# Moving the first expert's weight split into the last chunks of the block loop, with a new order for the last second products and for one 2 MB load

## The reference

```python
kv  = softmax(k, over tokens).T @ v                     # per batch and head
x   = softmax(q, over channels) @ kv                    # [4608, 512]
h   = x @ w_in                                          # [4608, 2048]
y   = (h - tanh(h)) @ w_out                             # [4608, 512]
logits = norm(y) @ norm(expert_emb).T / tau             # 8 experts
e, gate = argmax(logits), softmax(logits)[argmax]
out = gate * (relu(y @ w1[e]) @ w2[e])                  # w1 512x1024, w2 1024x512 for each expert
```

## Time and profile before

| what | value |
|---|---|
| time before, median of 3 runs | 1449.97 us (1447.04 to 1451.49) |
| the profiled execution's own time | 1449.26 us |
| its span, first to last instruction | 1447.2 us |
| mean granted TensorE clock | 0.998 of full |
| block loop ends, expert loop begins | about 967 us from the span's start |
| DMA over the span | 90.58 MB, mean 63 GB/s |

### The profile page before, as it was taken

How to read it: one execution, slowest core, us unless ns; L and a number is a source line. 1 busy time by engine, 2 the same in 40 slices (tenths; PEclk the granted TensorE clock), 3 DMA queues, 4 the chain that set the end, 5 groups by cost and what they waited for, 6 DMA issues and landing times.

```text
span 1447.2 us, 27386 instructions
## 1 busy us (share of the span) xinstructions
PE 1413.6 (98%) x8120; PEld 1218.9 (84%) x8121; DVE 904.7 (63%) x1755; ACT 765.1 (53%) x1574; POOL 396.6 (27%) x346
## 2 busy tenths in 40 slices
PE   6999999999999999999999999999999999999997
PEld 5788888888888888888888888878788888888886
DVE  7986788886688888578888666676314213342111
ACT  5886576666666676657666666663313223242211
POOL 4522253433244443325343323231000000000000
PEclk9999999999999999999999999999999999999999
DMA  9631021221011222002121002035411411411110
GB/s 214 179 93 61 1 72 30 68 50 49 1 47 43 55 50 50 25 1 72 30 68 26 23 1 81 0 103 192 136 44 61 139 44 40 160 36 46 44 38 29
DMA packets 140226, 90.58 MB, mean 63 GB/s; under 512 B 116504, under 2 KB 120856, under 8 KB 139936
## 3 DMA queue, kind: packets, MB, share of 16 engines
q1 hardware_dynamic: 133344, 69.27, 18.5%
q0 software_dynamic: 5840, 18.92, 3.4%
q10 hardware_dynamic: 880, 0.55, 0.1%
HBM read 69.80 MB, written 21.28 MB: 63 GB/s over the span
## 4 chain that ended last, share of the span: by engine, by line
PE 88%; DVE 5%; issue 2%; ACT 2%; DMA 1%; POOL 1%; ACTq 0%; SPq 0%; DVEq 0%; POOLq 0%
PE ps L554 26%; PE ps L555 26%; PE ps L556 25%; PE ps L632 2%; PE ps L752 2%; PE ps L654 1%; PE ps L724 1%; PE ps L643 1%; PE ps L638 1%; DVE gs L1054 1%; PE ps L674 1%; PE ps L625 1%; DMA out<-osb,xrow 1%; PE ps L597 1%; DMA xrow<-scratch 1%
## 5 line engine op out<-in xcount | busy, mean ns | idle before, releaser
L1461 POOL TENSOR_TENSOR g_lo<-gs,g_hi 128x384 fp32r<-128x384 f32 x192 | 199.0, 1037 | 575.4 <-ACT g_hi L851 575.2
L554 PE MATMUL ps<-x_hi,wi_hi 128*128 128x384 f32 x768 | 277.9, 362 | 2.2 <-DVE x_lo L1108 1.1
L555 PE MATMUL ps<-x_lo,wi_hi 128*128 128x384 f32 x768 | 260.0, 339 | 0.0
L556 PE MATMUL ps<-x_hi,wi_lo 128*128 128x384 f32 x768 | 259.9, 338 | 0.0
L841 ACT ACTIVATE usq<-ps 128x384 f32<-128x384 f32 x192 | 94.1, 490 | 290.4 <-PE ps L556 289.8
L554 PE MATMUL ps<-wo_hi,g_hi 128*128 128x512 f32 x576 | 228.4, 397 | 4.4 <-POOL g_lo L1461 3.0
L555 PE MATMUL ps<-wo_lo,g_hi 128*128 128x512 f32 x576 | 229.1, 398 | 0.0
L556 PE MATMUL ps<-wo_hi,g_lo 128*128 128x512 f32 x576 | 227.4, 395 | 0.0
L965 ACT ACTIVATE hb<-ps 128x512 f32<-128x512 f32 x74 | 44.3, 599 | 308.4 <-PE ps L556 303.9
L1051 DVE SCALAR_TENSOR_TENSOR gs<-gs,ps 128x384 f32<-128x384 f32 x192 | 105.8, 551 | 152.0 <-ACT gs L846 151.4
L1054 DVE TENSOR_TENSOR gs<-gs,usq 128x384 f32<-128x384 f32 x192 | 176.7, 920 | 0.0
(11 more groups left out here) (213 smaller groups left out, 2682.0 us busy)
## 6 DMA issues: line engine op xcount, KB each, us to landing
w_raw<-w SPq DMA_DIRECT2D x10, 2048.0 KB, 9.0
xrow<-scratch SPq DMA_DIRECT2D x36, 257.0 KB, 2.7
k_sb<-k SPq DMA_DIRECT2D x60, 144.0 KB, 3.4
q_sb<-q SPq DMA_DIRECT2D x60, 144.0 KB, 3.0
v_sb<-v SPq DMA_DIRECT2D x60, 144.0 KB, 3.4
in_raw<-w_in SPq DMA_DIRECT2D x8, 512.0 KB, 6.8
out_raw<-w_out SPq DMA_DIRECT2D x8, 512.0 KB, 6.0
scratch<-pad_d SPq DMA_DIRECT2D x8, 257.0 KB, 4.4
```

The source lines that it names most:

```text
L554: mm(out_, a_hi, b_hi, start=first, stop=False)
L555: mm(out_, a_hi, b_lo, start=False, stop=False)
L556: return mm(out_, a_lo, b_hi, start=False, stop=last)
L1461: G.tensor_tensor(g_lo[:, (s - 1) % 3], gs[:, (s - 1) % 2], g_hi[:, (s - 1) % 3].bitcast(F32), ALU.subtract).then_inc(glo_ready, 1)
```

## The change

Five edits go together. (1) The first expert's w1 is split by column halves: piece 0 is columns 0 to 511 of all four rows, piece 1 the rest (`first_piece`, `first_raw`). The left half is split inside the loop: ACT's copy ahead of slot 43 (`SUPER - 5`), and the subtraction on DVE in two parts of 128 x 1024, ahead of slots 43 and 45 (`left_lo`); it raises `left_ready`, on which alone `hidden(0, half 0)` waits. The right half's copy stands ahead of slot 46. (2) The second products of the last two chunks issue the six passes on `g_hi` first and wait for `g_lo` only then. (3) `g_lo` of the very last chunk is computed by DVE (`last_lo`). (4) The last-but-one block's third scatter is issued in the same slot as the other two, and so ahead of `g_lo` of chunk 46 on POOL. (5) SP issues the load of w2 only when the rows of 11 blocks are stored.

```diff
--- before.py
+++ after.py
@@ -291,7 +291,7 @@
     first_step, first_known, second_known, tab_step, tab_ready, pads_stored = (
         sem(x) for x in ("first_step", "first_known", "second_known", "tab_step", "tab_ready", "pads_stored"))
     raw_in = [sem("w1_raw_in"), sem("w2_raw_in")]
-    b_hi_done, w_ready = sem("b_hi_done"), sem("w_ready")
+    b_hi_done, w_ready, left_ready = sem("b_hi_done"), sem("w_ready"), sem("left_ready")
     row_in = [sem(f"row_in{i}") for i in range(4)]
     out_stored = [sem(f"out_stored{i}") for i in range(4)]
     t_ready, thi_ready, tlo_ready, hid_ready, relu_done = (
@@ -379,6 +379,17 @@
         if i < 2:
             return w1_raw[:, 2 * i:2 * i + 2].rearrange("p c n -> p (c n)")
         return w2_raw[:, 4 * (i - 2):4 * (i - 1)].rearrange("p c n -> p (c n)")
+
+    def first_piece(w_1, w_2, i):
+
+        if i < 2:
+            return w_1[:, 0, :, 512 * i:512 * (i + 1)]
+        return w_2[:, 0, 4 * (i - 2):4 * (i - 1)]
+
+    def first_raw(i):
+        if i < 2:
+            return w1_raw[:, :, 512 * i:512 * (i + 1)]
+        return w2_raw[:, 4 * (i - 2):4 * (i - 1)]
 
     def startup(engine, part, chunk_, piece_, emb_):
 
@@ -488,6 +499,7 @@
         row0 = sp.value_load(e_row[0:1, 0:1], min_val=0, max_val=ROWS - KNOWN * P)
         for j in range(KNOWN):
             sp.dma_start(xrow[:, j], scratch[ds(row0 + j * P, P), :]).then_inc(row_in[j], 16)
+        sp.wait_ge(rows_stored, 16 * GPB * (NBLK - 1))
         load_w2(e0)
 
         def entry(t, col, hi):
@@ -575,6 +587,18 @@
             c = s % FC1
             if isinstance(m, int) and m == 0 and s < FC1 and s % 2 == 0:
                 pe.wait_ge(wo_lo_done, s // 2 + 1)
+            if isinstance(m, int) and m * SUPER + s >= NCH - 2:
+                pe.wait_ge(ghi_ready, done(m, s))
+                for g in range(GPB):
+                    t = slice(g * P, (g + 1) * P)
+                    mm(y_ps[g], g_hi[:, s % 3, t], wo_hi[:, c], start=False, stop=False)
+                    mm(y_ps[g], g_hi[:, s % 3, t], wo_lo[:, c], start=False, stop=False)
+                pe.wait_ge(glo_ready, done(m, s))
+                for g in range(GPB):
+                    t = slice(g * P, (g + 1) * P)
+                    last = mm(y_ps[g], g_lo[:, s % 3, t], wo_hi[:, c], start=False, stop=c == FC1 - 1)
+                last.then_inc(l2_done, 1)
+                return
             pe.wait_ge(glo_ready, done(m, s))
             for g in range(GPB):
                 if c == 0:
@@ -735,6 +759,9 @@
 
             if hf == 0:
                 pe.wait_ge(tlo_ready, t + 2)
+            if isinstance(t, int) and t == 0 and hf == 0:
+                pe.wait_ge(left_ready, 1)
+            elif hf == 0 or isinstance(t, int) and t == 0:
                 pe.wait_ge(w_ready, e * 2 + 1)
             pe.wait_ge(relu_done, t * 2 + (hf + 1))
             f = slice(512 * hf, 512 * (hf + 1))
@@ -932,17 +959,16 @@
         def hi_of_first(i):
 
             act.wait_ge(raw_in[i // 2], 16)
-            nc.scalar.copy(expert_piece(w1_hi, w2_hi, i, 0), expert_raw(i)).then_inc(b_hi_done, 1)
+            if i < 2:
+                act.wait_ge(h_ready, done(3, SUPER - 5 + 4 * i))
+            nc.scalar.copy(first_piece(w1_hi, w2_hi, i), first_raw(i)).then_inc(b_hi_done, 1)
 
         def t_split(t, j):
             act.wait_ge(t_ready, t + 1)
             nc.scalar.copy(t_hi[:, j % 2], ps[:, 0].rearrange("p (c n) -> p c n", c=DC)).then_inc(thi_ready, 1)
 
-        def first_hi():
-            t_split(0, 0)
-            hi_of_first(1)
-
-        walk(act, slot, {SUPER - 2: lambda: hi_of_first(0), SUPER - 1: first_hi})
+        walk(act, slot, {SUPER - 5: lambda: hi_of_first(0), SUPER - 2: lambda: hi_of_first(1),
+                         SUPER - 1: lambda: t_split(0, 0)})
 
 
 
@@ -1238,10 +1264,27 @@
         def lo_of_first(i):
 
             dve.wait_ge(b_hi_done, i + 1)
-            last = V.tensor_tensor(expert_piece(w1_lo, w2_lo, i, 0), expert_raw(i),
-                                   expert_piece(w1_hi, w2_hi, i, 0).bitcast(F32), ALU.subtract)
+            last = V.tensor_tensor(first_piece(w1_lo, w2_lo, i), first_raw(i),
+                                   first_piece(w1_hi, w2_hi, i).bitcast(F32), ALU.subtract)
             if i % 2:
                 last.then_inc(w_ready, 1)
+
+        def left_lo(b):
+
+            dve.wait_ge(b_hi_done, 1)
+            d = slice(2 * b, 2 * b + 2)
+            last = V.tensor_tensor(first_piece(w1_lo, w2_lo, 0)[:, d], first_raw(0)[:, d],
+                                   first_piece(w1_hi, w2_hi, 0)[:, d].bitcast(F32), ALU.subtract)
+            if b == 1:
+                last.then_inc(left_ready, 1)
+
+        def last_lo():
+
+            c = SUPER - 1
+            dve.wait_ge(glo_ready, done(3, c, -1))
+            dve.wait_ge(ghi_ready, done(3, c))
+            V.tensor_tensor(g_lo[:, c % 3], gs[:, c % 2], g_hi[:, c % 3].bitcast(F32),
+                            ALU.subtract).then_inc(glo_ready, 1)
 
         e_used, e_turn, e_below, e_is, e_other, e_no = (x[:] for x in early)
         one_e = cst[0:1, C_ONE:C_ONE + 1].broadcast_to([1, E])
@@ -1267,7 +1310,7 @@
             V.tensor_copy(e_first[:], e_used[:, 0:1])
             V.tensor_scalar(e_row[:], e_used[:, 0:1], float(REGION), float(P), ALU.mult, ALU.add).then_inc(first_known, 1)
 
-        walk(dve, slot, {EARLY: choose_first})
+        walk(dve, slot, {EARLY: choose_first, SUPER - 5: lambda: left_lo(0), SUPER - 3: lambda: left_lo(1)})
         def t_split(t, j):
             dve.wait_ge(thi_ready, t + 1)
             V.tensor_tensor(t_lo[:, j % 2], ps[:, 0].rearrange("p (c n) -> p c n", c=DC),
@@ -1279,7 +1322,7 @@
                 V.tensor_tensor(h_lo[:, j % 2, 4 * b:4 * b + 4], ps[:, 3 + b].rearrange("p (c n) -> p c n", c=4),
                                 h_hi[:, j % 2, 4 * b:4 * b + 4].bitcast(F32), ALU.subtract).then_inc(hlo_ready, 1)
 
-        lo_of_first(0)
+        last_lo()
         t_split(0, 0)
         lo_of_first(1)
         route_part("tail_squares", NBLK - 1, 0)
@@ -1456,7 +1499,7 @@
 
         def lo(m, s):
 
-            if within(m, s, -1):
+            if within(m, s, -1) and not (isinstance(m, int) and m * SUPER + s == NCH):
                 pool.wait_ge(ghi_ready, done(m, s, -1))
                 G.tensor_tensor(g_lo[:, (s - 1) % 3], gs[:, (s - 1) % 2], g_hi[:, (s - 1) % 3].bitcast(F32),
                                 ALU.subtract).then_inc(glo_ready, 1)
@@ -1482,8 +1525,18 @@
                 if g == 0:
                     pool.wait_ge(dest_ready, j + 1)
                     hold(pool)
-                G.indirect_dma_start(scratch, bass.IndirectOffsetOnAxis(ap=dest[:, g:g + 1].bitcast(U32), axis=0),
-                                     yrow[:, g], None).then_inc(rows_stored, 16)
+                if isinstance(j, int) and j == NBLK - 2:
+                    if g == 1:
+                        scatter(1)
+                        scatter(2)
+                    elif g == 0:
+                        scatter(0)
+                else:
+                    scatter(g)
+
+        def scatter(g):
+            G.indirect_dma_start(scratch, bass.IndirectOffsetOnAxis(ap=dest[:, g:g + 1].bitcast(U32), axis=0),
+                                 yrow[:, g], None).then_inc(rows_stored, 16)
 
 
         def embeddings(i):
```

## The result

The changed kernel takes 1453.7 us in the median of 8 runs (1452.28 to 1454.79), the kernel before 1450.34 (1447.04 to 1452.12). The ratio is 1.0025, 95% interval 1.0015 to 1.0034: 3.4 to 3.6 us slower, inside the range and on the side that was forecast (+2.0). The span of the profiled execution is 1450.8 us, 3.6 more than before.

A forecast was written before the change was run, and what follows sets the result against it. PE was taken as the bound, busy 1413.6 of 1447.2 us. -2.95 (stalls gone) +3.6 (new wait) +1.3 (clock) = +1.95, say +2.0, on the median 1450.0 gave 1452.0 us; range 1447.3 to 1456.0.

The forecast's parts named there:

- Parts 1 to 3: Chunk 46 to hidden(0, half 0): halves cost nothing, new pass order and g_lo on DVE remove three stalls, -2.95 us.
- The scatters: POOL's scatters beside DVE's left parts: delay taken as 0, at most 0.8 us.
- The scatter's landing: Third scatter, from 958.58: lands after 4.8 us at 963.4, and only then SP issues w2.
- Part 4, the new wait: Before tail_logits: w2 takes 9.0 us, ACT's copies come late, PE idles 3.6 us, logits start 0.65 later.
- Part 5, the clock: At the 24 logits products: clock falls earlier after the idle time, some run at 1.2 GHz, +1.3 us.
- the recovery: Clock's recovery after the logits products: taken as nothing, bounds -1.4 to +0.7 us against before.
- Half of the bound: Clock cost in the logits products: bounds 0 and 2.7 us, of which half less a little was taken.
- What is absorbed later: Row load behind the table, PE's wait at 998.77: absorbs up to 0.55 us of what only PE loses.
- C: Logits: idle PE drops to 1.2 GHz before all 24 products, through hidden(1, half 0); +4.05, 1454 to 1457 us; chance 0.18.
- A: Before the logits: scatter and w2 land early, wait 0 to -2.1, clock around 0; 1448 to 1450.5 us; chance 0.22.
- B: ACT's wait off the path, w2 landed by 968.8: full gain -2.95 or -4.35, 1445.6 to 1447 us; chance 0.05.
- D: Last chunks: halves don't fit or POOL is held up, +0.8 us, 1452.8; chance counted within the forecast's 0.55.

The follow-up runs named there:

- e8: Changed kernel with both DVE left parts ahead of slot 43; one execution at granted clock 0.95, 1455.63 us, not compared.
- e6: Kernel before with only the w1 column halves, the other four edits undone; 1451.59 us beside 1449.77, ratio 1.0009 to before.
- e3: Changed kernel with 16 extra unused 512-column products on PE ahead of tail_logits; 1451.98 us beside 1448.64, ratio 1.0021 to before.
- e1: Changed kernel without SP's wait before loading w2; 1450.36 us beside 1448.64, ratio 1.0013 to before.
- e2: Kernel before with only SP's wait before loading w2 added; 1452.96 us beside 1448.64, ratio 1.0027 to before.
- e5: e4 with SP's load of the second expert's w1 put behind the table; 1452.88 us beside 1449.77, ratio 1.0019 to before.
- e7: Kernel before with only ACT's relu and tail_yT copies moved ahead of hi_of_first(2); 1450.86 us beside 1449.77, ratio 1.0004.
- e10: e4's kernel run again, beside e9; 1449.23 us against 1450.43, ratio 0.9991 to before.
- e4: Changed kernel without SP's wait, with ACT's relu and tail_yT copies ahead of hi_of_first(2); 1447.75 us beside 1448.64, ratio 0.9992 to before.
- e9: e4 with 10 extra unused 512-column products on PE ahead of rows_T(3); 1448.89 us beside 1450.43, ratio 0.9992 to before.

## Why the prediction came out as it did

The mechanism was the forecast's. Its terms, by its own steps:

- **Parts 1 to 3**, forecast -2.95, measured -2.36 at `hidden(0, half 0)`. The left copy and the two parts fitted where they were put, at no cost to the chunks' own work. The missing 0.6 us is all at chunk 46: its last three passes start 0.27 us later than forecast, because POOL's scatter was held up, and from there to `rows_T(0)` it is 1.16 us where the sum has 0.7. g_hi and g_lo of chunk 47 came as said.
- **The scatters** are the step that was wrong. I let DVE's part cost POOL nothing, with 0.8 as the bound. It cost 0.54: in the changed kernel the scatter issued beside it ends 0.84 us behind DVE's operation, in e8 without it it takes 0.96 again. The hint stood in the earlier trace rows: before, the third scatter (960.05, 1.12 us) ends 0.85 us behind DVE's operation at 959.39, and of the 33 scatters inside the loop in that trace the 22 that run beside this DVE operation take 1.11 to 1.29 us and end 0.84 to 1.07 behind it, while the other 11 take 0.96. "0.96 to 1.12" was read as nearly nothing, but a longer DVE operation holds the scatter longer. I had followed the Trainium skill (SBUF — State Buffer, "Who interferes with whom"), which supposes that a two-input DVE operation leaves descriptor writing alone and marks that as inferred; here the measurement decides: the indirect DMA waits. The same page's rule for POOL's reads fits (g_lo of chunk 47 with DVE out of its way is 1.00 us in e6, 2.57 before). The DVE operation beside it in the kernel before, which the earlier trace rows don't show, and POOL's in e6:

```profile
961.17 2.29 DVE L1241 TENSOR_TENSOR w_lo<-w_raw,w_hi 128x2048 fp32r<-128x2048 f32 x1
```
```profile
963.11 1.00 POOL L1490 TENSOR_TENSOR g_lo<-gs,g_hi 128x384 fp32r<-128x384 f32 x1 [0.57 <-ACT g_hi L865]
```

- **The scatter's landing**: taken as 4.8 us, it was 6.1 (958.72 to 964.83). With the 0.5 this is the 1.8 us by which w2 was issued later than forecast; w2 itself took 8.5, not 9.0.
- **Part 4, the new wait**: forecast 3.6 us, +0.65 at the logits; measured 4.26 and +2.08. So the mis-sized term is this one, by 1.4 us at the logits: 1.8 from w2's later issue, less 0.5 for its quicker transfer, and 0.1 between the landing and the products. The smaller gain doesn't move the logits; it brings PE to them 0.8 us later than forecast, and so the wait is only 0.7 longer.
- **Part 5, the clock**: forecast +1.3, measured +1.74 in the 24 products and nothing in the recovery (`hidden(1, half 0)` 4.4 us in both). e3 shows that it is the wait's doing: with PE busy until the logits they take 2.85 us. But the clock fell behind the start of the products, not ahead of it, and the cost doesn't follow the wait's length: 1.49 us of wait went with 4.59 us for the products (e6), 2.19 with 4.33 (e1), 2.28 with 3.03 (e2). Half of the bound was a guess that came near.
- **What is absorbed later**: the text allowed 0.55 us. At the ranks the changed kernel is 3.82 us late, at rows_T(3) 3.74, at tile 6 only 2.35. The kernel before waits there, and the changed one, already late, doesn't:

```profile
1021.60 0.66 PE L724 MATMUL ps<-ident,xrow 128*128 128x128 f32 x4 [0.40 <-DMA xrow<-scratch]
1023.01 0.49 PE L554 MATMUL ps<-w_hi,t_hi 128*128 x1 [0.75 <-issue]
```

So +2.0 was near +2.35 by luck, for two errors of opposite sign: too little at the logits (1.9 us), too little given back behind them (1.5). Between tile 6 (+2.35) and the end (+4.0 from R) the profiled execution loses another 1.6 us: its clock falls once more, some 12 us before its end, as it does in e3, e5, e7 and e10 but not in before, e1, e2, e4, e6 and e9. e4 and e10 are the same kernel, so this fall comes and goes from one execution to the next; from tile 6 to the end it is 387.9 to 388.5 us without it and 389.4 to 390.3 with it. The median over 8 runs, +3.4, has more than the 2.35; whether such falls are more frequent after the change (the mean granted clock of its runs is 0.9953, that of before beside the experiments 0.9973 to 0.9979) or this is chance was not settled, so about 1 us of the slowdown has no cause shown.

Of the rivals, C (the clock, late scatter, 1454 to 1457) has the result just below its lower end; its late scatter came true, its clock only in part, for that was 1.00 when the logits started and the recovery cost no more than before; A and B are out, because w2 never landed in under 8.5 us from its issue, and beside the scatters it took 11.2 (before) to 12.9 (e4); D happened in its POOL half.

The gain of the halves is real (2.3 us at `hidden(0, half 0)`, e6) and is lost in three places one behind the other: w2's landing in ACT's order (e1, e4), DVE's list behind it (e4), and the load of rows behind the table, slowed by w1 (e5). The first and the third were tested by an edit; the second is read from the traces of e4 and e7, and DVE's reading of the logits ahead of its subtraction for w2 was not run. No single edit tried here won it all; e4 (and e10, the same kernel) is the best found, 0.9 to 1.3 us under before, at the edge of what can be measured or below it, and by the ratios 4.8 us under the changed kernel.

## What to carry to other kernels

Before freeing an engine that is 98% busy, list what it will meet next and how early that is: here the copies were there 1.3 us ahead, so with ACT's order as it was, more than 1.3 us of gain could not pass. A load put off to spare the queue must be priced at its consumer, and in a strictly ordered list a wait for it holds everything behind it: put what the busy engine needs ahead of it. And a new wait of TensorE ahead of small products can cost more than its length: here the clock added 1.7 us at the logits, though most of what filling the wait won there was absorbed by the chain over the table (e3). Price each loss at the next place where the engines meet, not where it arises.

## What the runs showed of the hardware

- POOL's indirect DMA instruction takes 0.96 us alone and 1.50 beside a 128 x 1024 two-input subtraction on DVE, ending 0.84 us behind it (e8 against the changed kernel). In the trace of before it takes 1.11 to 1.29 beside the loop's 128 x 384 two-input operation, and ends 0.84 to 1.07 behind that one.
- w2's 2 MB took 8.5 to 9.7 us from issue to landing when issued behind the scatters (changed kernel, e3, e2), and 11.2 to 12.9 beside them (before, e1, e4); a scatter's landing varied from 3.3 to 7.5 us.
- 24 products of 8 columns took 2.74 us at a granted clock of 1.00 and up to 4.59 us where it fell among them (e6): the clock counts for such small products too.
- The clock's falls differ between executions of one kernel: behind the logits it fell in e10 and not in e4, which are the same code.
